# Attention and two feed-forward layers on one core: GpSimd's work in attention in another order

## What is computed

```python
def _attn_ref(q, k, v):                      # 4 batches, 8 heads, 576 positions, depth 64
    k_p = k.reshape(B, H, Sp, pool, D).mean(axis=3)      # keys pooled by 8: 72 a head
    v_p = v.reshape(B, H, Sp, pool, D).mean(axis=3)
    scores = scale * np.matmul(q, k_p.transpose(0, 1, 3, 2))
    scores = scores - np.max(scores, axis=-1, keepdims=True)
    attn = np.exp(scores)
    attn = attn / (np.sum(attn, axis=-1, keepdims=True) + 1e-09)
    return np.matmul(attn, v_p)

def _moe_ref(x, w_gate, w_val, w_out, rms_g):            # 2304 tokens, 512, 1536
    rms = np.sqrt(np.mean(x * x, axis=-1, keepdims=True) + 1e-06)
    xn = x / rms * rms_g
    g = xn @ w_gate
    silu = g * (1.0 / (1.0 + np.exp(-g)))
    return silu * (xn @ w_val) @ w_out

def _moe2_ref(x, w_in, w_out):                           # 2304 tokens, 512, 2048
    h = x @ w_in
    return (h * (1.0 / (1.0 + np.exp(-h)))) @ w_out
```

## Time and profile before

| | us |
|---|---|
| median of 3 runs | 890.89 |
| lowest and highest | 890.53, 891.65 |
| the profiled execution | 891.64 |
| its span in the profile | 889.90 |
| PE busy | 876.1, 98% |
| DVE, ACT, POOL busy | 505.9, 342.4, 265.5 |

### The profile page before, as it was taken

The page is one execution under the profiler, slowest core; times in us unless marked ns, Lnnn a source line. Parts: engine busy times, 40 slices in busy tenths (PEclk is TensorE's granted clock), DMA queues, the critical chain, the costliest instruction groups (busy, mean ns, idle before and its releaser), DMA issues.

```text
span 889.9 us, 12918 instructions
## 1 busy us (share of the span) xinstructions
PE 876.1 (98%) x4938; PEld 833.7 (94%) x4938; DVE 505.9 (57%) x845; ACT 342.4 (38%) x656; POOL 265.5 (30%) x281
## 2 busy tenths in 40 slices
PE   7999999999999999999999999999999999999998
PEld 7889999999999999999898999999998998989897
DVE  6678668776545666655654256665555454434433
ACT  4578834443222322346553222322234333322222
POOL 5798789885100002667772000000000000000000
PEclk9999999999999999999999999999999999999999
DMA  9962557778865552656779575555545545474321
GB/s 274 290 153 69 194 229 284 284 284 306 358 233 209 197 200 80 220 199 245 284 303 372 187 271 201 204 211 213 213 177 197 186 171 188 174 279 177 130 95 71
DMA packets 55740, 191.67 MB, mean 215 GB/s; under 512 B 21888, under 2 KB 32128, under 8 KB 42624
## 3 DMA queue, kind: packets, MB, share of 16 engines
q1 hardware_dynamic: 55680, 190.85, 59.7%
HBM read 134.74 MB, written 56.10 MB: 214 GB/s over the span
## 4 chain that ended last, share of the span: by engine, by line
PE 88%; POOL 5%; issue 3%; DMA 2%; DVE 1%; ACT 1%; SPq 0%; POOLq 0%; ACTq 0%; DVEq 0%
PE ps L1243 16%; PE ps L1245 16%; PE ps L1244 16%; PE ps L1309 7%; PE ps L1310 7%; PE ps L1308 7%; PE ps L1284 6%; PE ps L1283 6%; PE ps L1282 6%; DMA qs<-in_q 1%; POOL kv L527 1%; DMA kv<-in_k 1%; PE ps L1317 1%; PE ps L1177 1%; POOL rstd L608 1%
## 5 line engine op out<-in xcount | busy, mean ns | idle before, releaser
L1243 PE MATMUL ps<-xh,wr 128*128 128x384 f32 x840 | 282.2, 336 | 1.2 <-POOL wr L582 0.9
L1245 PE MATMUL ps<-xh,wr 128*128 128x384 f32 x840 | 281.3, 335 | 0.0
L1244 PE MATMUL ps<-xl,wr 128*128 128x384 f32 x840 | 281.0, 335 | 0.0
L1243 PEld LDWEIGHTS ps<-xh,wr 128*128 128x128 f32 x840 | 157.7, 188 | 4.2 <-POOL wr L582 1.5
L1244 PEld LDWEIGHTS ps<-xl,wr 128*128 128x128 f32 x840 | 157.7, 188 | 0.9
L1245 PEld LDWEIGHTS ps<-xh,wr 128*128 128x128 f32 x840 | 157.7, 188 | 0.0
L1310 PE MATMUL ps<-wo,al 128*128 128x512 f32 x288 | 112.5, 391 | 0.0
L1309 PE MATMUL ps<-wo,ah 128*128 128x512 f32 x288 | 112.4, 390 | 0.0
L1308 PE MATMUL ps<-wo,ah 128*128 128x512 f32 x288 | 112.0, 389 | 0.0
L1029 DVE TENSOR_TENSOR xacc<-ps,xacc 128x384 f32<-128x384 f32 (+1 forms) x102 | 62.4, 612 | 81.4 <-PE ps L1284 50.5
L747 ACT ACTIVATE ah<-qt 128x384 fp32r<-128x384 f32 x96 | 44.9, 517 | 139.5 <-PE ps L1310 126.5
(11 more groups left out here) (131 smaller groups left out, 1152.8 us busy)
## 6 DMA issues: line engine op xcount, KB each, us to landing
wr<-ring_home SPq DMA_DIRECT2D x40, 1792.0 KB, 7.3
ring_home<-wr SPq DMA_DIRECT2D x20, 1792.0 KB, 8.1
wo<-out_home SPq DMA_DIRECT2D x28, 1024.0 KB, 4.8
out_home<-wo SPq DMA_DIRECT2D x14, 1024.0 KB, 9.1
raw_c<-in_moe_w_out SPq DMA_DIRECT2D x13, 512.0 KB, 7.1
qs<-in_q SPq DMA_DIRECT2D x16, 256.0 KB, 4.8
kv<-in_k SPq DMA_DIRECT2D x3, 1024.0 KB, 6.9
kv<-in_v SPq DMA_DIRECT2D x3, 1024.0 KB, 8.6
```

The source lines that it names most:

```text
L1243: pe.matmul(out_ps, w_hi, x_hi, start=first and c == 0, stop=False, skip_group_check=True)
L1244: pe.matmul(out_ps, w_hi, x_lo, start=False, stop=False, skip_group_check=True)
L1245: ins = pe.matmul(out_ps, w_lo, x_hi, start=False, stop=c == 1, skip_group_check=True)
```

## The change

- Rstd of tiles 0 and 1 is made inside the summing of batch 1: tile 0 after its keys, tile 1 after its values.
- The sums of batch 3 start a tile later and keep one piece a tile: keys at POOL's tile 7 (before 6) and 8, values at 9 (before 8) and 10, value blocks after rstd(11) (before after rstd(10)). For batch 2 the places stay.
- The four sums of weight 0 are split: two behind the value blocks of batch 2, two behind those of batch 3. Its low parts stand at tiles 12 and 13 (before all at 11), the sums of weight 1 at 14 (before 12), `out_low` at 15 (before 14), the first two low parts of weight 1 at 16 and the rest after the tiles (before all after the tiles).
- On ACT, the third high part of weight 0 moves from tile 10 to 13 and the copy of wo from 13 to 14. `weight_high` waits for the sums only ahead of its third operation.
- SP loads the first raw weight after q(7) and the second after q(11) (before both after q(6)), keys of batch 3 after q(8) and its values after q(10) (before both after q(8)).
- The transposes of x(16) stand behind group 3 of unit 0, and DVE's write of it behind its second combination. `WARM` is 30.

```diff
@@ -33,7 +33,7 @@
     FF1, FF2 = w_gate.shape[1], w2_in.shape[1]
     E = D + 1
     HB = H // 2
-    WARM = 36
+    WARM = 30
     H0 = [c * P // SP for c in range(RC)]
     HN = [(min((c + 1) * P, R) - 1) // SP - H0[c] + 1 for c in range(RC)]
     HS = max(HN)
@@ -435,12 +435,10 @@
                 load_q(n)
                 if n in (4, 5):
                     load_kv(2, n - 4)
-                if n == 6:
-                    load_raw(made_at["r", 0])
-                    load_raw(made_at["r", 1])
-                if n == 8:
-                    load_kv(3, 0)
-                    load_kv(3, 1)
+                if n in (7, 11):
+                    load_raw(made_at["r", n // 11])
+                if n in (8, 10):
+                    load_kv(3, n // 10)
                 if n == 13:
                     for m in EARLY:
                         load_raw(made_at[m])
@@ -549,7 +547,7 @@
                                    vmask8[:, :, :].unsqueeze(3).broadcast_to([P, RC, HS, D]), ALU.mult)\
                     .then_inc(s_vb, 1)
 
-            def weight_sums(i):
+            def weight_sums(i, halves=(0, 1)):
                 u = made[i][1]
                 r = raw[raw_of(i)][:, :].rearrange("p (c n) -> p c n", c=KC)
                 a11, a12, a21, a22 = r[:, 0:2, 0:P], r[:, 2:4, 0:P], r[:, 0:2, P:2 * P], r[:, 2:4, P:2 * P]
@@ -561,26 +559,31 @@
                 if u == 2:
                     pool.wait_ge(s_o, NT)
                 pool.wait_ge(s_raw[raw_of(i)], 16 * raw_count[i])
-                pool.tensor_tensor(s1, a21, a22, ALU.add).then_inc(s_ws, 1)
...
+                if 0 in halves:
+                    pool.tensor_tensor(s1, a21, a22, ALU.add).then_inc(s_ws, 1)
+                    pool.tensor_tensor(s3, a11, a21, ALU.subtract)
+                if 1 in halves:
+                    pool.wait_ge(s_ws, sums0[i] + 1)
...
-            def ring_low(i):
...
+            def ring_low(i, ops=(0, 1, 2)):
...
+                if 0 in ops:
+                    pool.wait_ge(s_whi, his0[i] + 1)
...
+                if 1 in ops:
+                    pool.wait_ge(s_whi, his0[i] + 2)
...
+                if 2 in ops:
+                    pool.wait_ge(s_whi, his0[i] + 3)
...
             def out_low(i):
                 w, r = wo[o_slot(made[i][1])], raw[raw_of(i)][:, :].rearrange("p (c n) -> p c n", c=2)
@@ -592,11 +595,7 @@
             pool_rest(0, 0, KPARTS[2][1])
             step(pool_pairs(0, 1, VPARTS[1][1], RC))
             pool_rest(0, 1, VPARTS[1][1])
-            for kind in (0, 1):
-                pool_pairs(1, kind, 0, 2)
-                step(pool_pairs(1, kind, 2, RC))
-                pool_rest(1, kind, 0)
-            for n in range(NT):
+            def mean_square(n):
                 pool.wait_ge(s_ss, n + 1)
                 if n >= 1:
                     pool.wait_ge(s_rstd, n)
@@ -606,25 +605,37 @@
                 if n >= 2:
                     pool.wait_ge(s_xn, n - 1)
                 pool.tensor_tensor(rstd[:, n % 2:n % 2 + 1], ms[:, :], half[:, :], ALU.pow).then_inc(s_rstd, 1)
+
+            for kind in (0, 1):
+                pool_pairs(1, kind, 0, 2)
+                step(pool_pairs(1, kind, 2, RC))
+                pool_rest(1, kind, 0)
+                mean_square(kind)
+            for n in range(2, NT):
+                mean_square(n)
+
                 for b in (2, 3):
                     for kind in (0, 1):
-                        if n == 4 * b - 6 + 2 * kind:
+                        if n == 5 * b - 8 + 2 * kind:
                             pool_pairs(b, kind, 0, 2)
                             step(pool_pairs(b, kind, 2, RC))
-                        if n == 4 * b - 5 + 2 * kind:
+                        if n == 5 * b - 7 + 2 * kind:
                             pool_rest(b, kind, 0)
-                    if n == 4 * b - 2:
+                    if n == 5 * b - 4:
                         value_blocks(b)
-                if n == 5:
-                    weight_sums(0)
-                if n == 11:
-                    ring_low(0)
+                        weight_sums(0, (b - 2,))
                 if n == 12:
+                    ring_low(0, (0, 1))
+                if n == 13:
+                    ring_low(0, (2,))
+                if n == 14:
                     weight_sums(made_at["r", 1])
-                if n == 14:
+                if n == 15:
                     out_low(made_at["o", 0])
-
-            ring_low(made_at["r", 1])
+                if n == 16:
+                    ring_low(made_at["r", 1], (0, 1))
+
+            ring_low(made_at["r", 1], (2,))
             for i in range(3, len(made)):
                 if made[i][0] == "r":
                     weight_sums(i)
@@ -667,13 +678,17 @@
                     return
                 w, t = wr[x % RING], wt[x % RING]
                 r = raw[raw_of(i)][:, :].rearrange("p (c n) -> p c n", c=KC)
-                act.wait_ge(s_ws, sums0[i] + 3)
+                if x >= RING:
+                    act.wait_ge(s_prod, NF * (x - RING + 1))
+                if x - RING in r_store:
+                    act.wait_ge(s_rst[x % RING], r_store[x - RING])
                 if 0 in ops:
                     act.activation(w[:, 0, 0:2, :, :].rearrange("p f c n -> p (f c) n"), r[:, :, 0:P], ACT.Copy)\
                        .then_inc(s_whi, 1)
                 if 1 in ops:
                     act.activation(w[:, 0, 2, :, :], r[:, 2:4, P:2 * P], ACT.Copy).then_inc(s_whi, 1)
                 if 2 in ops:
+                    act.wait_ge(s_ws, sums0[i] + 3)
                     act.activation(w[:, 0, 3:7, :, :], t[:, :, :, :], ACT.Copy).then_inc(s_whi, 1)
 
             def token_high(b, f):
@@ -842,9 +857,9 @@
                         norm(n - 2)
                     if n >= 1:
                         squares(n - 1)
-                    if n in (8, 9, 10):
-                        weight_high(0, (n - 8,))
-                    if n == 13:
+                    if n in (8, 9, 13):
+                        weight_high(0, ((8, 9, 13).index(n),))
+                    if n == 14:
                         weight_high(made_at["o", 0])
                     if n in (15, 16, 17):
                         weight_high(made_at["r", 1], (n - 15,))
@@ -1035,11 +1050,11 @@
                     low(n - 1, 2)
                     low(n - 1, 3)
                 combine_u2(x)
-                if x == 0:
-                    scale_x(NT - 2)
                 if prior == 1:
                     gate(x - 1, 3)
                 combine_u3(x)
+                if x == 0:
+                    scale_x(NT - 2)
                 if prior == 1:
                     low(n - 1, 1)
                     low(n - 1, 2)
@@ -1244,7 +1259,7 @@
                         pe.matmul(out_ps, w_hi, x_lo, start=False, stop=False, skip_group_check=True)
                         ins = pe.matmul(out_ps, w_lo, x_hi, start=False, stop=c == 1, skip_group_check=True)
                     ins.then_inc(s_prod, 1)
-                    if u == 0 and i == 2:
+                    if u == 0 and i == 3:
                         transpose_x(NT - 2)
 
             def perms_free(n):
```

More of the change, by code:

```diff
@@ L574, in ring_low @@
                 w, t = wr[u % RING], wt[u % RING]
-                pool.wait_ge(s_whi, his0[i] + 1)
-                pool.tensor_tensor(w[:, 1, 0:2, :, :].rearrange("p f c n -> p (f c) n"), r[:, :, 0:P],
-                                   w[:, 0, 0:2, :, :].rearrange("p f c n -> p (f c) n"), ALU.subtract)
-                pool.wait_ge(s_whi, his0[i] + 2)
-                pool.tensor_tensor(w[:, 1, 2, :, :], r[:, 2:4, P:2 * P], w[:, 0, 2, :, :], ALU.subtract)
-                pool.wait_ge(s_whi, his0[i] + 3)
-                pool.tensor_tensor(w[:, 1, 3:5, :, :], t[:, 0:2, :, :], w[:, 0, 3:5, :, :], ALU.subtract)
-                pool.tensor_tensor(w[:, 1, 5:7, :, :], t[:, 2:4, :, :], w[:, 0, 5:7, :, :], ALU.subtract)\
-                    .then_inc(s_wlo, 1)
+                if 0 in ops:
+                    pool.wait_ge(s_whi, his0[i] + 1)
+                    pool.tensor_tensor(w[:, 1, 0:2, :, :].rearrange("p f c n -> p (f c) n"), r[:, :, 0:P],
+                                       w[:, 0, 0:2, :, :].rearrange("p f c n -> p (f c) n"), ALU.subtract)
+                if 1 in ops:
+                    pool.wait_ge(s_whi, his0[i] + 2)
+                    pool.tensor_tensor(w[:, 1, 2, :, :], r[:, 2:4, P:2 * P], w[:, 0, 2, :, :], ALU.subtract)
+                if 2 in ops:
+                    pool.wait_ge(s_whi, his0[i] + 3)
+                    pool.tensor_tensor(w[:, 1, 3:5, :, :], t[:, 0:2, :, :], w[:, 0, 3:5, :, :], ALU.subtract)
+                    pool.tensor_tensor(w[:, 1, 5:7, :, :], t[:, 2:4, :, :], w[:, 0, 5:7, :, :], ALU.subtract)\
+                        .then_inc(s_wlo, 1)
             def out_low(i):
```

8 lines of the change are left out of this document (3 added, 5 removed).

## The result

The changed kernel takes 895.23 us, median of 5 runs (893.68 to 896.30), beside 890.69 us for the kernel before (5 runs, 890.25 to 891.65): a ratio of 1.0049, 95% interval 1.0034 to 1.0063. It is slower by 4.5 us. The forecast was 893.9 with a range of 889.6 to 896.6 and slower as the likeliest sign: the sign is right, the time is in the range, and the forecast is 1.3 us too low. That the number came so close is partly luck, since how often the clock falls in a run is chance, and the five runs reach from 893.7 without a fall to 896.3. The profiled execution took 896.09, its span is 894.4.

What follows compares the result with a forecast made beforehand. PE waits for nothing from 118 us on, so unit 2's start decides, set by earlier waits in attention's 18 tiles. Unit 2 +1.6 and one clock fall +1.4 sum to +3.0: 893.9 us on the 890.89 median, range 889.6 to 896.6.

Steps and rivals of the forecast that it cites:

- pv(3): Attention product of token tile 3 on PE (pv(n) is that of tile n): start 30.3 instead of 32.08, -1.8 us.
- pv(10): Tile 10's attention product: DVE's token sums take turns with POOL's K sums; start 62.9 against 64.96, -2.05, PE waits 2.2.
- pv(12): Tile 12's attention product: freed by DVE at 73.7 after turns with POOL's V sums of batch 3, -2.5 us.
- pv(13): Tile 13's attention product: waits 2.6 us for batch 3's value blocks, now behind rstd(11); start 80.5 against 80.36, +0.15.
- product 3: In unit 0: out_low between rstd(15) and rstd(16) delays norm(16); start 103.9 against 101.82, +2.1, PE waits some 2.7.
- The start: Warm-up: six fewer warming transposes end it 0.65 to 1.0 us earlier, lost in the wait for value blocks; value 0.
- Early rstd: Rstd of tiles 0 and 1 before batch 1's V sums: x(0) ready when PE gets there, -1.8 us.
- Loads: Raw weights and fourth keys and values no longer ahead of q(9), whose transposes wait 0.4: -0.4 us (0 to -0.5).
- The rival in which DVE comes first: DVE's operations start before POOL's sums or are let past, no wait long enough for the clock: 889.0 us, chance 0.12.
- ACT in tiles 13 and 14: Two copies of 1.04 us in neighbouring tiles, ACT having some 0.4 spare a tile: +0.4 us (0 to 0.7).
- Units 1 and 2: After unit 0: unit 1 at 109.1, +2.2; the wait before unit 2 goes, unit 2 at 116.7, +1.6 us.
- The clock and the base: One clock fall from three long waits, +1.4 us (0 to 3.4); sum put on the median of three, 890.89.

Runs made afterwards that it cites:

- the repeated run: The changed kernel run again unaltered, against the kernel before: median 895.29 us, ratio 1.0039, 11 runs; its profiled execution has no clock fall.
- the first two groups: Comparisons on one chip each, changed variants beside the kernel before, which took median 891.83 us in one (34 runs) and 891.53 in the other (28).
- the versions: Kernels keeping early rstd and moved loads, DVE's token sums later, against the kernel before: 889.40 us (POOL order kept), 889.05 (POOL reordered), 889.25 (reordered, 36 warming transposes).
- the kernel with the third wait filled: Changed kernel plus 22 unused identity transposes on PE ahead of product 3 of unit 0: median 894.46 us, ratio 1.0022 to the kernel before.

## Why the prediction was nearly right, and where it was not

Starts of PE, minus those of the kernel before. The last column is the execution of the changed kernel without a fall, both kernels counted from their own pv(0), because the start itself moves by a microsecond (below). The starts of the kernel before are those of its profile, with its fall, in every column.

| place | forecast | profile after | without a fall, from pv(0) |
|---|---|---|---|
| pv(3) | -1.8 | -1.67 | -1.82 |
| pv(9) | -2.25 | -1.85 | -1.51 |
| pv(10) | -2.05 | -1.86 | -1.52 |
| pv(12) | -2.5 | -1.96 | -2.15 |
| pv(13) | +0.15 | +0.28 | +0.46 |
| product 3 | +2.1 | +4.18 | +2.74 |
| unit 1 | +2.2 | +5.52 | +2.66 |
| unit 2 | +1.6 | +4.71 | +1.85 |

- **The start.** Fewer warming transposes were valued at nothing. Right, and for the reason given: in all 13 profiles pv(0) waits for the value blocks and starts 3.95 or 3.96 after POOL's first sum of V, with 36 transposes as with 30.
- **Early rstd.** -1.8 forecast, -1.67 and -1.82 measured. Right.
- **Loads.** -0.4 forecast. Half right. Eight profiles share this part of the changed kernel. In four of them pv(9) is 40.00 or 40.01 behind pv(0), against 42.26 before, and so 0.4 more than pv(3) has gained; in the other four it is 40.25 to 40.75, and in the execution of the last column (40.75) the gain is gone. Ahead of pv(9) single q loads are late by 0.4 to 1.1 in some executions and not in others, so a wait of 0.4 read from one trace is not a term to be counted on.
- **pv(10).** Right as a mechanism and in its place. rstd(7) was forecast from 56.3, and it stands at 56.53; the K sums from 57.1, and stand at 57.32; DVE was held as said, and PE waited 1.93 where 2.2 was forecast. The rival in which DVE comes first is dead: POOL began its sums 0.9 before DVE asked. The Trainium skill (SBUF, State Buffer, section "Who interferes with whom") has the order of issue decide who blocks. The rows agree operation by operation: POOL's first sum led, and DVE's 0.95 became 1.21; DVE's first was then ahead of POOL's second, and POOL's two sums took 3.77 for 3.04; DVE's second, behind POOL's second, took 2.58. A lead held for one operation and not for the pair.
- **pv(12).** Forecast 73.7 and released by DVE, measured 74.25 with no wait ahead of it: the fall behind pv(10) kept PE busy for longer, and DVE was done. Without a fall it is -2.15, with a short wait for DVE (the second of the two in the wait row of the repeated run).
- **pv(13).** +0.15 forecast, +0.28 measured, wait 2.6 forecast, 2.16 with a fall ahead of it and 2.56 without. Right, and shown by the kernel in which the blocks come earlier. The working has a small gap: 77.7, 0.85 and 1.80 add up to 80.35, so the step to 80.5 stands there without a source; the trace has 0.11 from the end of the blocks to pv(13).
- **ACT in tiles 13 and 14.** +0.4 forecast. Right: from pv(13) to pv(15) it is 9.55 without a fall, against 9.18 before.
- **Product 3.** +2.1 forecast with a wait of 2.7; the wait is 2.81. The start is +4.18 because the fall behind pv(13) lies ahead of it. Without a fall it is +2.74. norm(16) came at 104.10, where 101.6 to 102.2 was forecast; 1.6 of the lateness is that fall.
- **Units 1 and 2.** No wait ahead of unit 2, as forecast, and from unit 1 to unit 2 the time falls from 8.18 to 7.37.
- **The clock and the base, the step that failed.** The path without the new fall was forecast at +1.6 and measured, from pv(0), at +1.85, of which 0.75 arose before pv(9), most of it behind a q load that was 0.54 late; without it the path is +1.1. But one fall was forecast, at +1.4, and the changed kernel has 1.6 to 1.8 a run, three in its profile. And the kernel before has only 0.5: 37 of its 62 runs in the first two groups have none. The profile of before happened to be an execution with one, so every start that the sum subtracts from, from pv(12) on, holds that fall's 1.7 us, and leaving it out of the path after counts as a saving. The sum then added the result to the median of 890.89, which is most likely an execution without a fall (the clock of that run is not on record; the three groups have 891.2 to 891.5 for such runs). Put right, the sum is 890.9 + 1.6 + 1.5 = 894.0 with no fall after, where the one such run of the first five took 893.68 and the four of the repeated set took 893.81 on average on a base 0.3 higher. The run with the median time, 895.23, has a clock of 0.996, two falls by the count, and is 1.55 above the run without. That is the price of one: either one of the two cost nearly nothing, as the first did in the profile, or the runs differ by other things as well; without its trace this stays open. So the forecast left out 1.5 us at the base, and its one fall at +1.4 was about what two falls cost. The text had seen that the profiled execution lay 0.75 above the median, and carried the 0.75 over without asking what it was; its fall is the likely reason, though a fall is 1.5 and other things move a run as well.

## What to carry to other kernels

An operation of a helping engine that is shifted "one tile later" must be followed to its reader: here the value blocks, one tile later, ended 2 us behind the moment at which the matrix engine came for them, and `out_low`, one tile later, held up norm(16) and with it product 3 by nearly 3. Where two engines stretch each other's operations, find out which of them meet before and after the shift; moving two of them a tile was worth 1.3 us in the traces here and 1.7 in the run times. And before a profiled execution is used as base for a sum, compare its clock with that of the other runs: an event that only some executions have must be put in, or left out, on both sides.

## What was not expected of the hardware

- **A fall of the clock is a matter of chance at a given wait.** The same three waits of 1.9, 2.6 and 2.8 us brought no fall in one execution, and waits of 1.9, 2.2 and 2.8 brought three in another. What can be planned for is a mean number: 0.5 to 0.9 a run in the kernel before, 1.6 to 1.8 in the changed kernel with its three waits of 2 to 3 us, 0 to 0.3 in the versions. A long wait is not needed: the fall of the kernel before stands behind waits of 0.88 and 0.85.
- **A fall has no fixed price.** 1.6 and 1.4 where PE was then the bound, 0.2 where the next wait was due in any case.
- **The first load of V sets the start anew in each execution.** pv(0) starts between 16.35 and 17.72 over these profiles, and between 16.69 and 17.16 for one and the same kernel. POOL's first sum of V, which waits for its load, begins between 12.40 and 13.77, and pv(0) always follows 3.95 or 3.96 later. Not the wait for the first q tile: it is 0.3 and 1.2 in the two executions of the changed kernel, but only because the warming ended earlier in the second; the q transposes start 0.16 apart. POOL and PE of the kernel before, then of the kernel with the third wait filled:

```profile
12.57 1.27 POOL L527 TENSOR_TENSOR kv<-kv 128x512 f32<-128x512 f32 x1 [3.93 <-DMA kv<-in_v]
...
16.53 1.75 PE L1177 MATMUL ps<-vb,prT 128*128 128x130 f32 x12 [0.81 <-DVE vb L892]
```

```profile
13.77 1.27 POOL L525 TENSOR_TENSOR kv<-kv 128x512 f32<-128x512 f32 x1 [4.79 <-DMA kv<-in_v]
...
17.72 1.75 PE L1192 MATMUL ps<-vb,prT 128*128 128x130 f32 x12 [1.79 <-DVE vb L907]
```
